# Second column pair with eight plain products, row tiles for the second group's turns and q's product, identity products ahead of the data

## The reference

```python
kv = einsum('bhsd,bhse->bhde', k, v)          # q, k, v: batch 4, heads 8, 576 tokens, 64
out = einsum('bhsd,bhde->bhse', q, kv)
x = out / sqrt(mean(out * out, -1) + 1e-6) * g_norm   # then (2304 tokens, 512)
h = x @ w_in;  x = (h * sigmoid(h)) @ w_out           # 512 -> 2048 -> 512
out = ((x @ w_a) * (x @ w_b)) @ w_out2                # 512 -> 1536 -> 512
```

## Time and profile before

| | |
|---|---|
| median of three executions | 897.32 us |
| profiled execution | 897.5 us, span 895.7 us |
| PE busy | 868.0 us (97% of the span), 6582 matmul records |
| DVE, ACT, POOL busy | 520.8, 282.0, 626.3 us |
| granted TensorE clock, mean of the span | 0.999 of full |
| mean of one in the first 260 us | `flush1` 453 ns, `silu` 754, `g_rest` 752, `g_round` 642, scaling of `o_sb` from PSUM 548 |
| chain that ended last | PE 86%, DVE 7%, POOL 2%, issue 2% |

### The profile page before, as it was taken

The page is one execution under the profiler, slowest core; times in us unless marked ns, Lnnn a source line. Parts: engine busy times, 40 slices in busy tenths (PEclk is TensorE's granted clock), DMA queues, the critical chain, the costliest instruction groups (busy, mean ns, idle before and its releaser), DMA issues.

```text
span 895.7 us, 16996 instructions
## 1 busy us (share of the span) xinstructions
PE 868.0 (97%) x6582; PEld 821.9 (92%) x6582; DVE 520.8 (58%) x816; ACT 282.0 (31%) x470; POOL 626.3 (70%) x911
## 2 busy tenths in 40 slices
PE   7889999999999999999999999999999999999998
PEld 6678899999999999999989999999998999999996
DVE  2697575657887665556774454453573544545536
ACT  2764353434543322222432121121251221211210
POOL 1596446654597777775588687887979877777760
PEclk9999999999999999999999999999999999999999
DMA  9742232510011111111111011111110250111103
GB/s 269 177 101 75 67 62 56 120 47 26 27 45 48 48 49 48 49 48 48 33 40 48 25 48 50 46 48 48 48 48 25 84 140 24 52 48 44 48 25 106
DMA packets 47103, 55.63 MB, mean 62 GB/s; under 512 B 11952, under 2 KB 32432, under 8 KB 47024
## 3 DMA queue, kind: packets, MB, share of 16 engines
q1 hardware_dynamic: 44304, 49.55, 20.1%
q10 hardware_dynamic: 2720, 4.98, 1.9%
HBM read 49.81 MB, written 4.72 MB: 61 GB/s over the span
## 4 chain that ended last, share of the span: by engine, by line
PE 86%; DVE 7%; POOL 2%; issue 2%; ACT 1%; DMA 1%; SPq 0%; DVEq 0%; ACTq 0%; POOLq 0%
PE ps L734 45%; PE ps L798 7%; PE ps L799 7%; PE ps L800 7%; PE ps L820 5%; PE ps L822 5%; PE ps L821 5%; PE ps L691 2%; DVE x_lo L1290 2%; DMA kvq<-in_v_dram 1%; PE ps L665 1%; PE ps L701 1%; DVE g_lo L1358 1%; DVE o_sb L1249 1%; DVE ps L1336 1%
## 5 line engine op out<-in xcount | busy, mean ns | idle before, releaser
L734 PE MATMUL ps<-x_hi,w_hi 128*128 128x288 f32 x1092 | 236.5, 298 | 4.8 <-ACT kept L1038 2.4
L734 PE MATMUL ps<-x_lo,w_hi 128*128 128x288 f32 x1092 | 234.0, 296 | 0.0
L734 PE MATMUL ps<-x_hi,w_lo 128*128 128x288 f32 x1092 | 232.9, 295 | 0.0
L734 PEld LDWEIGHTS ps<-x_hi,w_hi 128*128 128x128 f32 x1092 | 179.1, 188 | 17.1 <-POOL w_lo L478 5.0
L734 PEld LDWEIGHTS ps<-x_hi,w_lo 128*128 128x128 f32 x1092 | 176.1, 189 | 0.0
L734 PEld LDWEIGHTS ps<-x_lo,w_hi 128*128 128x128 f32 x1092 | 174.7, 188 | 0.0
L476 POOL TENSOR_SCALAR w_hi<-wt 128x256 fp32r<-128x256 f32 x156 | 70.4, 451 | 129.4 <-PE ps L734 125.1
L798 PE MATMUL ps<-g_hi,d_hi 128*128 128x288 f32 x512 | 154.2, 301 | 3.2 <-DVE g_lo L1358 1.2
L1038 ACT COPY kept<-ps 128x576 f32<-128x576 f32 x117 | 75.1, 642 | 254.2 <-PE ps L734 253.4
L1372 DVE TENSOR_TENSOR xy<-xy,ps 128x288 f32<-128x288 f32 x224 | 100.8, 453 | 88.5 <-PE ps L800 87.5
L800 PE MATMUL ps<-g_hi,d_lo 128*128 128x288 f32 x512 | 150.9, 295 | 0.0
(11 more groups left out here) (104 smaller groups left out, 1211.4 us busy)
## 6 DMA issues: line engine op xcount, KB each, us to landing
raw<-in_moe_w_out_dram SPq DMA_DIRECT2D x28, 512.0 KB, 3.8
raw<-in_moe_w_in_dram SPq DMA_DIRECT2D x15, 512.0 KB, 3.5
raw<-in_moe_w_a_dram SPq DMA_DIRECT2D x12, 512.0 KB, 3.6
raw<-in_moe_w_b_dram SPq DMA_DIRECT2D x12, 512.0 KB, 3.5
kvq<-in_k_dram SPq DMA_DIRECT2D x12, 288.0 KB, 5.1
kvq<-in_v_dram SPq DMA_DIRECT2D x12, 288.0 KB, 6.6
out_dram<-xy SPq DMA_DIRECT2D x27, 128.0 KB, 2.4
kvq<-in_q_dram SPq DMA_DIRECT2D x16, 144.0 KB, 6.4
```

Of the source, the lines that this page charges most:

```text
L734: mm = pe.matmul(ps[:, bank + s, 0:PART], w, x[:, n, c, s * PART:(s + 1) * PART], start=(begins and first), stop=last, skip_group_check=no ...
```

## The change

1. Pair 1 too is done with eight plain products, so that pair 2 is the first that needs the sums. `SECOND_STEPS` goes; the second pair has its own table of products, tiles and banks, two down tiles after every product, and no `part` and no `add`. GpSimd splits the four quarters of its weights instead of making their sums.
2. The sums and the rests of operands 1, 2, 4 and 5 move out of pair 0's lists into pair 1's, on DVE, ACT and GpSimd; the rests of operand 4 into pair 2. s4 gets a place of its own (`held`).
3. Group 1's turns and q's product are done in row tiles of 64 partitions: a turn is 6 transposes of 64 rows by 128 into 64 columns instead of 3 of 128 by 128, q's product 12 matmuls of 64x64 with 64 columns instead of 6 with 128. The halves lie in banks 6 and 7, so each such slot takes both banks (`take_slot`), and the next down tile waits for the eviction whichever bank it has. ACT evicts from both banks with one instruction.
4. `WARM` becomes 12 identity matmuls ahead of group 0's first turns and 13 more behind them, ahead of its first `kv`.

```diff
-    SLOT_BANKS = (2, 1, 1, 1, 1, 1, 1, 0, 0, 1, 1, 1)
+    SLOT_BANKS = (2, 2, 2, 2, 2, 2, 2, 0, 0, 2, 2, 2)
...
+             ((0, 0, BANK_B, True), (3, 2, BANK_B, False), (0, 1, BANK_C, True), (3, 3, BANK_C, False),
+              (7, 0, BANK_A, True), (6, 2, BANK_A, False), (7, 1, BANK_B, True), (6, 3, BANK_B, False)))
...
-    SECOND_STEPS = (5, 3, 0, 1, 2, 4, 6)
+    PLAIN_PAIRS = 2
+    PLAIN_TILES_AFTER = 2
-    WARM = 9
+    WARM = (12, 13)
...
+            def turn_batches(src):
+                for n in range(3):
+                    for bb in range(2):
+                        rows = slice(bb * HALF, (bb + 1) * HALF)
+                        mm = pe.transpose(ps[:, BANK_D + bb, n * HALF:(n + 1) * HALF], src(n)[rows], ident[rows, rows])
+                return mm
+
+            def take_slot(sem, count):
+                wait_turn(BANK_D)
+                wait_turn(BANK_D + 1)
+                turn[BANK_D] = turn[BANK_D + 1] = (sem, count)
...
+            def q_kv1(h, j):
+                i = UNITS + JS * h + j
+                pe.wait_ge(qT_kept, i + 1)
+                pe.wait_ge(kv_kept, PAIRS + h + 1)
+                take_slot(o_kept, i + 1 - UNITS)
+                for n in range(3):
+                    for odd in range(2):
+                        rows = slice(odd * HALF, (odd + 1) * HALF)
+                        for bb in range(2):
+                            at = bb * TILE3 // 2 + n * HALF
+                            mm = pe.matmul(ps[bb * HALF:(bb + 1) * HALF, BANK_D + odd, n * HD:(n + 1) * HD],
+                                           qT_sb[rows, i % 3, at:at + HALF], kv_sb[rows, h % 2, bb, rows],
+                                           start=True, stop=True)
+                mm.then_inc(o_mm, 1)
...
+            def second_pair():
+                t = 0
+                for k in range(len(PLAIN[1])):
+                    if PLAIN[1][k][3]:
+                        pe.wait_ge(g_ready, (g_count(0, 3), g_count(0, 1), g_count(0, 2), g_count(1, 0))[k // 2])
+                    plain_half(1, k, 0)
+                    if k < STEPS:
+                        attend(STEPS + k)
+                    plain_half(1, k, 1)
+                    for _ in range(PLAIN_TILES_AFTER):
+                        down1(0, t)
+                        t += 1
...
-            for _ in range(WARM):
-                pe.matmul(ps[:, BANK_D, 0:P], ident[:], ident[:], start=True, stop=True)
+            warm(WARM[0])
             for j in range(JS):
-                q_turn(0, 0, j, first_bank(0, j))
+                q_turn(0, j, first_bank(0, j))
+            warm(WARM[1])
             kv(0, 0)
```

More of the change, by code:

```diff
@@ L515, in second_up, with second_split @@
             def second_up():
[L516 to L532, removed]
+                quarter = quarters(1)
+                def second_split(at):
+                    w = PLAIN_SLOT.index(at)
+                    pool.wait_ge(prod, after(0, max(k for k in range(8) if PLAIN[0][k][1] == w)))
+                    split(RING + at, at, quarter[w])
+                second_split(0)
+                second_split(1)
+                half_sum(5, 0)
+                half_sum(5, 1)
+                second_split(2)
+                second_split(3)
+                half_sum(1, 0)
+                half_sum(2, 0)
             def head_pairs():
@@ L693, in q_kv, with o_turn @@
                 mm.then_inc(o_mm, 1)
-                turn[bank] = (o_kept, i + 1 - UNITS) if G else (n_ready, i + 1)
-            def o_turn(G, h, j, bank):
-                i = UNITS * G + JS * h + j
+                turn[bank] = (n_ready, i + 1)
+            def o_turn(h, j, bank):
+                i = JS * h + j
                 pe.wait_ge(n_ready, i + 1)
@@ L737, in half, with plain_half @@
                     mm.then_inc(prod, 1)
[L739 to L753 removed]
+            def plain_half(pp, k, c):
+                n, w, bank, begins = PLAIN[pp][k]
+                at = PLAIN_SLOT[w]
+                if c == 0:
+                    pe.wait_ge(w_ready, w + 1 if pp == 0 else RING + at + 1)
+                if pp == 0:
+                    pe.wait_ge(*x_split(0, n, c))
+                hi, lo = w_hi[:, at, c, :], w_lo[:, at, c, :]
+                for w_part, x, first, last in ((hi, x_hi, c == 0, False), (hi, x_lo, False, False),
+                                               (lo, x_hi, False, c == 1)):
+                    for s in range(2):
+                        mm = pe.matmul(ps[:, bank + s, 0:PART], w_part,
+                                       x[:, x_place(n), c, s * PART:(s + 1) * PART],
+                                       start=(begins and first), stop=last, skip_group_check=not begins)
+                if c == 1:
+                    mm.then_inc(prod, 1)
+            def plain(k):
+                plain_half(0, k, 0)
+                plain_half(0, k, 1)
             def may_begin(u, n):
@@ L894, in layer2, with warm @@
                 down2(pp - 1, 8)
+            def warm(count):
+                for _ in range(count):
+                    pe.matmul(ps[:, BANK_D, 0:P], ident[:], ident[:], start=True, stop=True)
             pe.wait_ge(consts, 3)
-            for _ in range(WARM):
-                pe.matmul(ps[:, BANK_D, 0:P], ident[:], ident[:], start=True, stop=True)
+            warm(WARM[0])
             for j in range(JS):
-                q_turn(0, 0, j, first_bank(0, j))
+                q_turn(0, j, first_bank(0, j))
+            warm(WARM[1])
             kv(0, 0)
@@ L915, in _ @@
             for j, bank in enumerate((2, 6, 7)):
[L916 removed]
+                o_turn(3, j, bank)
             pe.wait_ge(n_ready, UNITS)
@@ L919, in _ @@
             first_pair()
-            for pp in range(1, PAIR0[-1]):
+            second_pair()
+            for pp in range(PLAIN_PAIRS, PAIR0[-1]):
                 if SEGS[seg_of(pp)][1] == 1:
@@ L931, in _, with square @@
         def _(act):
-            def square(G, h, j, bank):
+            def square(G, h, j, bank=None):
                 i = UNITS * G + JS * h + j
```

265 lines of the change are left out of this document (129 added, 136 removed).

## The result

| | before | changed |
|---|---|---|
| median (lowest to highest) of 20 executions each | 897.79 us (895.17 to 899.60) | 899.61 us (897.03 to 900.45) |
| ratio | | 1.0023, 95% interval 1.0014 to 1.0031 |
| profiled execution, its span | 897.5, 895.7 us | 899.35, 897.5 us |
| mean granted clock of the profiled span | 0.999 | 0.996 |

The change made the kernel 0.23% slower, where 894.1 us was forecast, inside 888.5 to 898.5. The mechanisms of the early stages came as forecast, and more than was won there was lost in pairs 2 to 6.

What follows compares the result with a forecast made beforehand. TensorE was taken as full from about 100 us, with DVE late in pair 0 and a slow clock at the start. Terms -2.7 - 4.0 + 1.6 - 2.3 + 0.6 - 0.6 + 1.4 + 2.8 = -3.2 gave 894.1 us; range 888.5 to 898.5.

Steps and rivals of the forecast that it cites:

- start: Before the first plain product: more identity products raise TensorE's clock before 9 us, first `o_sb` turn near 20.2; -2.7 us.
- pair 0: Sums and rests leave pair 0, so TensorE's waits on DVE's `x_lo` and `g_lo` go; -4.0 us.
- pair 1 and start of pair 2, without their turns: One more product +1.6, fewer waits in pair 1 -2.3, later q-turn eviction starting pair 2 +0.6 us.
- q's product, nine: Row tiles save 0.40 us a slot, then about 0.33 waiting for `o_sb`: -0.07 in nine slots, -0.6 us.
- Row tiles, the turns: Turns from pair 1 on: a slot costs 0.40 us, +0.07 in 21 slots, +1.4 us; bounds -3.4 and +11.
- a rival in which it stays low until 14.6 us: At the start, TensorE stays at 1.2 GHz, delaying the first k'v product; 1.9 us of gain lost, 896.0 us; chance 0.10.
- Both banks: Pairs 3 to 6: late ACT evictions in step 5, 3 x 0.7, and two longer flush waits, 2 x 0.36; +2.8 us.
- The start of pair 2: Pair 2's first product: q-turn eviction behind `g_hi` and `x_hi` on ACT makes PE wait 1.8 us; +0.6 us.
- What was won comes back at the banks: Turns: rounds at 0.109 make a slot 0.53 us, 2.7 us more in all, 896.8 us; chance 0.16.
- Tiles nearly free: Turns cost 0.17 us each, 0.056 a round without drain; 4.8 us less, 889.3 us; chance 0.20.
- turns run in sequence: A turn's two row tiles don't overlap: slot 0.86 us, 9.7 us more, 903.8 us; chance 0.12.

Runs made afterwards that it cites:

- `warm_only`: The kernel before with only the 12 and 13 identity products in place of 9: 894.77 us, ratio 0.9974.
- `both_banks`: `full_turns`, but each turn takes both banks though it writes only one: 901.45 us, ratio 1.0053 to the kernel before.
- `full_turns`: The changed kernel with group 1's turns as three 128x128 transposes in one bank again, q's product still in row tiles: 892.83 us, ratio 0.9955 to the kernel before.
- `rows_fixed`: The changed kernel with two moves, ACT's eviction of pair 2's first turn and a DVE scaling in pair 2 earlier: 896.22 us, ratio 0.9986 to the kernel before.
- `turns_twice`: The changed kernel with each turn's three rounds issued twice, same values to the same place: 901.83 us in one execution, slot 0.72 us.
- `pair_only`: The kernel before with only the eight-product second pair and moved sums and rests, nine identity products, no row tiles: 892.7 us, ratio 0.9956.
- `rows_only`: The kernel before with only row tiles for group 1's turns and q's product, both banks held: 904.93 us, ratio 1.0091.

## Why the prediction was wrong, step by step

The steps of the sum in the changed kernel:

| step | forecast | measured |
|---|---|---|
| start | -2.7 | -1.7 with a fall of the clock in it; -3.25 in `warm_only`, which had none |
| pair 0 | -4.0 | -3.3, with three turns in it that I had not counted (+0.6), and q's products at +0.5 instead of +0.15 |
| pair 1 and start of pair 2, without their turns | -0.1 | -0.65 - 5 x 0.20 = -1.6 |
| q's product, nine | -0.6 | 9 x (-0.31 + 0.24 + 0.08) = +0.1 |
| turns, 21 from pair 1 on | +1.4 | 21 x 0.20 = +4.2 |
| both banks, from pair 2 on | +2.8 | +2.4 |
| clock | 0 | 2 falls in most executions, some 1.3 us each; about one of them new |

*The failed step is "Row tiles, the turns".* I took 3 x 0.067 + 0.20 = 0.40 for a turn. The rounds were right (0.058 to 0.065), the way in and out was not: 0.35, not 0.20. The mistake can be seen in the earlier trace rows. I divided q's slot of 1.00 into 0.80 of product (208.70 - 207.90) and 0.20 of entry, but the 0.80 runs up to the next product's first matmul and so holds the way out as well. At 0.109 for each of six rounds the product itself is 0.65 and the rest 0.35. In q's product, which pays the way in and out in both kernels, the same slip made the saving 0.40 where it was 0.31; the wait came 0.09 shorter than I had it (0.24 for 0.33), and that the two cancel is luck. For the turns, which had none, it was the whole price: 0.13 us in 21 slots, 2.7 us, with 3 x 0.20 more in pair 0, whose turns I left out of the sum.

A caution goes with this. The 0.52 is the price inside the slot. By `both_banks`, full turns would have saved only 0.4 us as long as both banks were held (201.41 - 1.7 against 199.34). What the forecast had as two terms, +1.4 and +2.8, is one thing, the turns in row tiles with both their banks; it measured 7.2 us with pair 0's (4.2 + 0.6 + 2.4), and 7.25 as the difference to `full_turns` from the first plain product on, without the clock's 1.7.

The Trainium skill ("TensorEngine Tiling (Array Packing)", Tiling Modes) says that a change of the tiling mode drains TensorE. The trace agrees, and puts 0.35 us on a change and the change back; that it is a drain which takes this time no row shows. The prediction quoted the rule and then priced it from a row that held only part of it.

*The second failure is a term that was missing: the clock.* I had a rival in which it stays low until 14.6 us; that did not happen (the k'v product ran 1.28 us at 11.40). Instead it rose, as forecast, and fell again at 20.2 and at 122.6. An execution without any fall took 897.0, one with both 899.6. By `rows_fixed` the second most likely hangs on the waits in pairs 2 and 3, of which one grew from 0.64 to 1.30 us and one from 1.5 to 1.85, where the turn now waits for one flush more. That price of holding both banks was not in the sum. What makes the first fall stays open.

Between the profiled executions the sum should have been -3.2 and was +1.85, 5.05 us more: the turns 2.7, those of pair 0 another 0.6, the two stretches at half clock 2 x 3.4 / 2 = 3.4 us (about 1.3 each by the medians of whole executions), and -1.7 for everything else: the start beside its fall 0.7 and pair 1 with the start of pair 2 1.6 less than forecast (no wait is left in pair 1, where I had allowed 0.5, and at the start of pair 2 it is 1.46 for 1.8; 0.7 of the 1.6 I can't assign), the banks 0.4 less, q's nine products 0.7 more, and small change.

*Both banks* came near the forecast in the changed kernel, in part by luck. Late evictions in step 5 of pairs 3, 4 and 6 (two of them on `xy` and one on `qT_sb`) cost 0.41, 0.52 and 0.50 us in distances between matmuls, and the 0.08 behind each; forecast were 3 x 0.7. An `o_sb` in pair 5, which was not forecast, was 0.37 later than its sisters. The two `o_turn`s behind a flush came 0.37 and 0.18 later, of which 0.10 each is the way into the tiles and stands in the turn's price already; forecast were 0.36 each. That is 2.4. With the 16 turns (3.1), the clock (1.7) and q's products (0.1) it makes the 7.3 us of the fourth stretch.

*The start of pair 2* came as forecast in kind: ACT's eviction stands behind the last `g_hi` and `x_hi` of operand 4, and TensorE waited 1.46 us; the forecast was 1.8. `full_turns` has the same queue on ACT and waits nothing at that tile, since the other bank lets it through, and 0.7 us one tile later. The kernel before waited 0.64 us there. So this wait, which I put down to the second pair alone, needs the held banks too.

*The rivals.* "What was won comes back at the banks" named a slot of 0.53 us and 896.8 in all. The slot is 0.52, and the execution without a fall took 897.0. But its reason, rounds at 0.109, is refuted by `turns_twice`: 3 x 0.109 + 0.20 and 3 x 0.058 + 0.35 come to the same by accident. "Tiles nearly free" falls with `full_turns`, "turns run in sequence" with the 0.40 us of the six records (one after the other they would need 6 x 0.11). The Trainium skill's remark (same page, Performance Considerations) that tiling does not speed up the emptying of PSUM holds in q's product: 0.31 us less on TensorE were followed by 0.24 of waiting for ACT, and 0.08 more behind the wait.

## What to carry to other kernels

Price a small operation between others by the distance between its neighbours' starts, with it and without it, and not by its own row: what it costs to change the tile shape and back (0.35 us here) lies outside the row, and is as large as three transposes. In the slot, row tiles gained 0.31 us in q's product, which had paid for a change of tile before, and lost 0.20 in the turns, which had not. And a second bank held for them gives the gain back as soon as the eviction is the later of the two, and for q's product all of it went that way. Before blaming one of two things that came together, take it away alone: with both banks still held, giving up the turns' row tiles gained next to nothing. And look behind a wait of one to two microseconds for a fall of the clock, which costs about as much again; it follows in some executions and not in others.

## What the runs showed of the hardware that was not expected

- Leaving 128x128 tiles for 64-row tiles and coming back cost 0.35 us, whether k'v's (1.40 us for 18 rounds), q's product (0.70 for 6) or a turn (0.52 for 3) stood between. A round, in which up to four tiles work side by side, took 0.058 us at full clock, a full transpose or a pair of 128x64 tiles 0.109.
- A down tile that had to wait for its bank went on more slowly once: its second matmul started 0.21 us behind the first instead of 0.13. In `both_banks` this came 19 times more often than in `full_turns`, 1.5 us that no row of idle time shows.
- The granted clock fell to half for 3.4 us at a time in some executions of a kernel and not in others; a fall cost about 1.3 us. Of the places where profiled executions show it (20.2 and 122.6 us in the changed kernel, 20.0 in `both_banks`, 31.1 in `pair_only`, 128.0 in `rows_only`, and, inside the second layer, beginning between 669 and 683 us in five kernels) only the one in pair 3 was traced to a wait, and there by counting executions; what decides in which execution it falls stays open. Filling idle time at the start with products may have made it rarer and did not end it.
